# Attention, MLP and experts on one core: MLP units one step sooner, low part of x ahead of the masks, low halves of the weights a step behind the high ones

## The reference

```python
# q, k, v: (4, 8, 576, 64)
scores = scale * q @ k.T;  kth = the 32nd largest of each row
attn = softmax(where(scores >= kth, scores, -1e9)) @ v      # 2304 tokens x 512
h = x @ w_in                     # x: (2304, 512), w_in: (512, 2048)
r = np.maximum(h, 0.0)
x = (r * r) @ w_out              # w_out: (2048, 512)
# then 8 experts, the best one per token where x @ w_skip > 0:
out = x + gate * (relu(x @ w1[e]) @ w2[e])
```

## Time and profile before

| | |
|---|---|
| median of 3 runs | 1019.26 us (1017.67 to 1019.67) |
| the profiled execution's own time | 1019.29 us |
| its span, first to last instruction | 1017.6 us |
| PE, DVE, ACT, POOL busy | 90%, 73%, 55%, 61% of the span |
| mean granted TensorE clock | 0.948 |

### The profile page before, as it was taken

How to read it: one execution, slowest core, us unless ns; L and a number is a source line. 1 busy time by engine, 2 the same in 40 slices (tenths; PEclk the granted TensorE clock), 3 DMA queues, 4 the chain that set the end, 5 groups by cost and what they waited for, 6 DMA issues and landing times.

```text
span 1017.6 us, 18907 instructions
## 1 busy us (share of the span) xinstructions
PE 920.3 (90%) x6160; PEld 696.1 (68%) x6161; DVE 743.5 (73%) x1609; ACT 563.4 (55%) x1183; POOL 623.2 (61%) x889
## 2 busy tenths in 40 slices
PE   3565589999999999999999999999999569999996
PEld 1343478888888888888888888888889444444442
DVE  6999989999999998999999999999300331111111
ACT  3666667776786777786777777777532101011010
POOL 2887878877787776887787887887744110101100
PEclk9866699999999999999999999999999759999998
DMA  8853334643554568656346446444376550724730
GB/s 321 330 178 108 112 111 126 202 161 116 189 173 134 187 224 247 201 174 195 132 146 194 149 130 204 138 137 128 122 234 263 208 206 21 286 102 168 274 127 5
DMA packets 66622, 174.56 MB, mean 172 GB/s; under 512 B 18450, under 2 KB 23570, under 8 KB 62176
## 3 DMA queue, kind: packets, MB, share of 16 engines
q1 hardware_dynamic: 64688, 168.35, 49.0%
q0 software_dynamic: 1840, 5.04, 1.6%
HBM read 153.63 MB, written 20.71 MB: 171 GB/s over the span
## 4 chain that ended last, share of the span: by engine, by line
PE 84%; POOL 5%; DVE 3%; ACT 3%; issue 3%; DMA 1%; SPq 0%; POOLq 0%; ACTq 0%; DVEq 0%
PE psum L934 8%; PE psum L1092 8%; PE psum L1075 8%; PE psum L914 7%; PE psum L974 7%; PE psum L976 7%; PE psum L975 7%; PE psum L991 7%; PE psum L992 6%; PE psum L993 6%; PE psum L953 6%; PE psum L917 2%; POOL w_in_low L503 2%; PE psum L1014 2%; POOL w_ring L496 1%
## 5 line engine op out<-in xcount | busy, mean ns | idle before, releaser
L765 DVE MAX8 top<-left 128x8 f32<-128x576 f32 x432 | 304.7, 747 | 0.0
L468 POOL TENSOR_TENSOR s_sb<-s_sb,below 128x576 f32<-128x576 f32 x144 | 204.4, 1424 | 46.4 <-ACT below L604 45.7
L771 DVE MATCH_REPLACE8 left<-top,left 128x576 f32<-128x576 f32 x288 | 211.7, 743 | 0.0
L974 PE MATMUL psum<-x_high,w_in_high 128*128 128x256 f32 x576 | 168.6, 293 | 0.6 <-ACT relu L637 0.6
L976 PE MATMUL psum<-x_high,w_in_low 128*128 128x256 f32 x576 | 163.4, 284 | 0.0
L975 PE MATMUL psum<-x_low,w_in_high 128*128 128x256 f32 x576 | 163.3, 283 | 0.0
L483 POOL TENSOR_TENSOR square<-relu 128x256 f32<-128x256 f32 x144 | 88.5, 615 | 91.7 <-ACT relu L637 91.7
L595 ACT ACTIVATE s_sb<-psum 128x576 f32<-128x576 f32 x144 | 93.5, 649 | 87.4 <-PE psum L914 71.3
L914 PE MATMUL psum<-k_sb,q_sb 64*128 64x288 f32 x512 | 109.3, 507 | 35.7 <-ACT s_sb L595 30.5
L604 ACT ACTIVATE below<-s_sb,steep_kth 128x576 f32<-128x576 f32 x144 | 110.8, 769 | 35.0 <-POOL neg_max L456 35.0
L488 POOL TENSOR_TENSOR g_low<-square,g_high 128x256 fp32r<-128x256 f32 x144 | 105.7, 734 | 25.9 <-POOL square L483 18.2
(11 more groups left out here) (150 smaller groups left out, 1449.7 us busy)
## 6 DMA issues: line engine op xcount, KB each, us to landing
w_ring<-w_split SPq DMA_DIRECT2D x144, 512.0 KB, 4.7
weights<-w SPq DMA_DIRECT2D x32, 1024.0 KB, 7.1
v_sb<-v_main SPq DMA_DIRECT2D x48, 256.0 KB, 2.6
w_split<-w_ring SPq DMA_DIRECT2D x16, 512.0 KB, 3.1
k_sb<-kT SPq DMA_DIRECT2D x32, 144.0 KB, 4.8
k_sb<-kT SPq DMA_DIRECT2D x32, 128.0 KB, 4.7
q_sb<-qT SPq DMA_DIRECT2D x32, 128.0 KB, 4.4
weights<-w_out SPq DMA_DIRECT2D x1, 4096.0 KB, 13.0
```

The costliest lines, as they stand in the source:

```text
L468: nc.gpsimd.tensor_tensor(s_sb[:, s % SBUFS, n, 0:S], s_sb[:, s % SBUFS, n, 0:S], below[:, n, :], ALU.subtract).then_inc(masked, 1)
L765: v.max(top[:, par, n, r, :], src).then_inc(topk_step, 1)
L771: v.match_replace(left[:, n, :], top[:, par, n, r, :], src, LOWEST).then_inc(topk_step, 1)
L974: t_.matmul(dst, wh, x_high[:, j % 2, k, :], start=k == 0, stop=False)
```

## The change

Four places: units begin at t = 10 and not 11 (`FIRST`), so that all of `ENDS` and `TIMES` move by one; POOL computes `x_low` ahead of the masks; the low halves of w_out come one t later (and so do SP's stores); the high halves of w_in come two t later and their low halves three.

```diff
-    FIRST = PER_GROUP + 3
+    FIRST = PER_GROUP + 2
...
 # SP
-                for f in split_parts(t, 0):
+                for f in split_parts(t - 1, 0):
                     sp.wait_ge(out_high, f + 1)
                     sp.wait_ge(out_low, f + 1)
...
 # POOL
                     normalise(t - 2, 1)
+                if 0 <= t - 3 < NS:
+                    split_x(t - 3)
                 if 0 <= t - 1 < NS:
                     mask(t - 1, 0)
                     mask(t - 1, 1)
-                if 0 <= t - 3 < NS:
-                    split_x(t - 3)
                 for u in slots:
                     square_low(u)
-                for f in split_parts(t, 0):
+                for f in split_parts(t - 1, 0):
                     split_out_low(f)
-                for f in split_parts(t, FT):
+                for f in split_parts(t - 3, FT):
                     split_in_low(f)
...
 # ACT
-                for f in split_parts(t, FT):
+                for f in split_parts(t - 2, FT):
                     split_in_high(f)
```

## The result

The changed kernel takes 1024.77 us (median of 4 runs, 1024.33 to 1026.2), the kernel before 1019.37 us (median of 4, 1017.67 to 1019.67). The ratio is 1.0059, with a 95% interval of 1.0041 to 1.0076: slower by 5.4 us. The profiled execution of the changed kernel is its slowest, 1026.2 us with a span of 1024.5 us.

The account below looks back on a forecast made before the run. PE was taken to pace the middle at 9.39 us a step, so the first 16 steps decide. +11.05 (step 16) - 5.64 + 1.10 (tail) = +6.5 us on 1019.3 gives 1025.8 us, range 1016.5 to 1031.

Parts of the forecast that it names:

- PE sets the middle, so the first 16 steps decide: Middle: PE paces 9.39 us a step without holes, so the +11.05 us at step 16 should reach the end.
- The start-up is freed: Steps 2 to 9: without POOL's 1.76 us wait DVE sets 9.70 us; step 10 begins at 106.33, -6.47 us.
- The low halves behind the units: Steps 10 to 14: POOL's w_in low halves, 3.72 us per three, 2.49 per two, make steps of 13.09, 14.00 (three times), 12.77.
- The clock's 1.52 us in each such step: Steps with units after idle PE: matmuls at 1.2 GHz take 4.43 us instead of 2.91, kept in each step.
- The rival of the clock at 2.4 GHz: Steps 11 to 15: PE's clock stays up, 6.97 us less, 1018.8 us in all; chance 0.16.
- Step 15 like step 12 of before: Step 15 has no low halves but follows an idle PE, so it takes 10.28 us.
- POOL's waits vanish: Rival, steps 10 to 15: POOL finds operands ready, steps 10 to 13 take 11.38 us; 1012.7 us in all; chance 0.12.
- The tail: End of MLP: one unit-pair step leaves, -5.64 us; the last group's wait for x_low adds +1.10 us.
- `split_x`: POOL's x_low ahead of the masks: hidden by 0.5 us in a full step, so up does not wait.
- Too late in every group: Each group's start: x_low computed behind the masks would come too late for up; no size given.
- DVE's idle time: Before DVE's reciprocals in the steps with low halves behind units: about 13 us in all.
- SyncE's stores: Stores move with the low halves, costed at nothing; without cover step 11 would wait 3.1 us for one landing.

Follow-up runs that it names:

- Experiment 7: Kernel before with low halves of both weights one step behind their high ones, w_in's high ones at t - 1, units unmoved: 1020.76 us, 1.0008.
- Experiment 2: Changed kernel with the pieces of both weights back at the steps of before, on SyncE, ACT and POOL: 1017.47 us, 0.9985 of the kernel before.
- experiment 3: Changed kernel with both halves of w_in one step sooner: 1020.94 us, 1.0015 of the kernel before.
- experiment 8: Changed kernel with four weight pieces a step instead of three and w_in sooner: 1012.52 us with four low halves behind units, 1007.92 us with none.
- experiment 4: Changed kernel with unread matmuls added ahead of PE's transposes in steps 11 to 15: 1030.8 us with 24, 1021.2 us with 11.
- experiment 5: Changed kernel with split_x back behind the masks: 1055.14 us, 1.0348 of the kernel before.
- experiment 1: Changed kernel with its units back at step 11: 1025.55 us, 1.0063 of the kernel before.
- experiment 6: Kernel before with split_x ahead of the masks and nothing else: 1019.4 us, 1.0001.

## Why the prediction was right

It said 1025.8 us, within 1016.5 to 1031, and 0.69 for slower; it came to 1024.77 (the profiled execution to 1026.2, of which 1.1 us lies behind the MLP, where the prediction had no change). Step by step:

- **PE sets the middle, so the first 16 steps decide.** Right: +10.30 at step 16, +10.29 at the last `steep_kth`, and the table above.
- **The start-up is freed.** Step 10 begins at 106.51, predicted 106.33. Experiment 7 shows that the lag alone does it.
- **The low halves behind the units.** 12.99, 13.83, 13.83, 13.75, 12.48 against 13.09, 14.00 three times, 12.77: 77.21 with step 15 instead of 78.14. Experiment 2 shows that this is the whole loss, experiments 3 and 8 that it shrinks with the number of low halves behind units.
- **The clock's 1.52 us in each such step.** Measured 1.3 (experiment 4), 1.56 (experiment 3 beside the changed kernel) and some 1.5 (experiment 5). The rival of the clock at 2.4 GHz falls: the granted clock is 0.50 behind the gaps of steps 11 to 15. "TensorE: Matmul & The Clock Gate" (What's actually happening) in the Trainium skill, read strictly, would have given that rival; the trace of the changed kernel doesn't agree, with gaps of 2.8 to 3.0 us and one of 1.59.
- **Step 15 like step 12 of before.** 10.33 against 10.28, but by luck of the clock: in the traces of experiments 1, 2, 3, 5 and 7 the step behind the last low halves took 8.75 to 8.78. Had it done so here, the profiled execution would have been 1.6 us shorter. The gap ahead of the transposes was 2.31 us in step 12 of before and 1.57 or 1.58 in these steps, so the row that was taken had the longer gap.
- **POOL's waits vanish.** They don't: in steps 10 to 14 of the changed kernel POOL works 55.5 of 66.9 us and waits the other 11.3, where this rival needed less than 6.6; even at full clock a step with three low halves takes 12.51 us, not 11.38. Without any low half the first steps came to 10.11 and 8.76 (experiment 8).
- **The tail.** -5.64 + 1.10 = -4.54 predicted, -4.50 measured, the wait for x_low 1.08.
- **`split_x`.** Hidden ahead of the masks, needed there: experiments 5 and 6. "Too late in every group" was right, and its price, not worked out in the prediction, is mostly 4 us a group and 30 in all.
- **DVE's idle time** was put at about 13 us, without a working, and is 16.1. It could have been worked out: from DVE's reciprocal at 116.03, the last without a wait, to the one at 181.22 are 65.2 us, and five times DVE's 9.70 taken from them leave 16.7.
- **SyncE's stores** were costed at nothing. No wait of PE, ACT, DVE or POOL on them shows from 20 to 190 us, but they were not tried apart from the rest.

## What to carry to other kernels

Work that is prepared for a later stage must be finished before that stage's engines fill up: on an in-order queue the same three low halves cost nothing while POOL rests and over 4 us a step behind the units. Taking a wait away by delaying its consumer moves the work as well, so ask where it lands before counting the wait as won; here both were had by preparing more pieces per step, with each low half one step behind its high one (1007.92 us). And a gap of PE is priced with what follows it: count the wait, and then the stretch at the lower clock.

## What the runs showed of the hardware

A single stop of 2.17 us in an otherwise full PE (8.00 of 8.00 us busy ahead of it) put the granted clock to 0.50 for the stretch behind it, and made a step longer by 4.0 us; in the same kernel a stop of 2.18 us left the clock at 1.00 and made a step longer by 2.4 us (experiment 5). Nearly equal gaps of 1.57 and 1.59 us, with the same instructions, left the clock at 1.00 in one kernel (experiment 3) and at 0.83 on average over the step in the other (the changed one). So the gap's length alone doesn't decide, and what does stays open. And an fp32 matmul of 128 columns stands in the trace as two instructions: 24 of them are 48 in 5.62 us, 0.117 us each at full clock.
